# Clearing a row buffer in two halves and reordering the first loads of an attention and feed-forward kernel

## What is computed

```
for t in range(S):
    cur = einsum('bhd,bhe->bhde', u * k[t], v[t])
    y[t] = einsum('bhd,bhde->bhe', r[t], state + cur)
    state = w * state + einsum('bhd,bhe->bhde', k[t], v[t])
x = y as (3072 tokens, 384)
h = x @ w_in;  x = (max(h, 0) + alpha * min(h, 0)) @ w_out
h = x @ w_in2; out = (h * tanh(log1p(exp(h)))) @ w_out2
```

## Time and profile before

| | |
|---|---|
| median of 3 runs | 1009.12 us |
| the runs | 1009.12, 1012.5, 1008.62 us |
| the profiled execution | 1010.13 us |
| its span in the trace | 1008.4 us |
| granted TensorE clock, mean | 0.999 of full speed |
| TensorE busy | 979.0 us, 97% of the span |
| VectorE, ScalarE, GpSimd busy | 660.3, 644.3, 374.2 us |

### The profile page before, as it was taken

One profiled execution on the slowest core, in us unless ns is written; L12 is line 12 of the kernel. 1 busy time (PEld: TensorE's weight loads), 2 busy tenths in 40 slices (PEclk: granted clock), 3 DMA queues, 4 the chain that ended last, 5 costly groups with the idle time before them and its releaser, 6 DMA issues.

```text
span 1008.4 us, 24355 instructions
## 1 busy us (share of the span) xinstructions
PE 979.0 (97%) x9476; PEld 801.9 (80%) x9476; DVE 660.3 (65%) x1421; ACT 644.3 (64%) x1456; POOL 374.2 (37%) x663
## 2 busy tenths in 40 slices
PE   4978999999999999999999999999999999999998
PEld 3866788888888887888878888888888888888886
DVE  6776776655655665665553345877768777777775
ACT  6765665545555555545554667877777777787775
POOL 7878776666656666655620340000000000000000
PEclk9999999999999999999999999999999999999999
DMA  5234341211121121111103232000000000000000
GB/s 171 65 84 130 108 123 51 86 45 45 46 78 47 53 76 44 51 55 61 29 6 134 90 94 95 32 1 32 32 32 7 26 31 0 0 31 0 32 1 31
DMA packets 24614, 54.33 MB, mean 54 GB/s; under 512 B 4928, under 2 KB 12736, under 8 KB 24512
## 3 DMA queue, kind: packets, MB, share of 16 engines
q1 hardware_dynamic: 22640, 43.43, 14.5%
q10 hardware_dynamic: 1872, 9.49, 2.3%
HBM read 41.10 MB, written 9.44 MB: 50 GB/s over the span
## 4 chain that ended last, share of the span: by engine, by line
PE 93%; DVE 2%; DMA 2%; SPq 1%; ACT 1%; issue 1%; POOL 0%; DVEq 0%; ACTq 0%; POOLq 0%
PE acc L979 41%; PE hid L963 29%; PE lev L963 10%; PE lev L1022 8%; PE tok L1040 2%; PE tok L1045 2%; DMA arena<-rk_t 2%; DVE scores L569 1%; SPq L304 1%; PE lev L1006 1%; ACT scores L819 0%; PE hid L1022 0%; PE acc L1040 0%; DVE w_lo L654 0%; DVE x_parts L587 0%
## 5 line engine op out<-in xcount | busy, mean ns | idle before, releaser
L963 PE MATMUL hid<-x_parts,w_hi 128*128 128x512 f32 x864 | 291.1, 391 | 3.6 <-DVE w_lo L654 3.6
L979 PE MATMUL acc<-g_hi,w_hi 128*128 128x512 f32 x576 | 233.2, 405 | 0.0
L979 PE MATMUL acc<-g_hi,w_lo 128*128 128x512 f32 x576 | 224.8, 390 | 0.0
L963 PEld LDWEIGHTS hid<-x_parts,w_hi 128*128 128x128 f32 x864 | 163.0, 189 | 38.1 <-issue 4.0
L660 DVE SCALAR_TENSOR_TENSOR hid<-relu_neg,neg_slope,hid 128x512 f32<-128x512 f32 x96 | 72.5, 756 | 170.0 <-ACT hid L856 169.8
L855 ACT ACTIVATE relu_neg<-hid 128x512 f32<-128x512 f32 x96 | 57.2, 596 | 197.6 <-PE hid L963 197.6
L963 PE MATMUL hid<-x_parts,w_lo 128*128 128x512 f32 x432 | 168.8, 391 | 0.0
L979 PE MATMUL acc<-g_lo,w_hi 128*128 128x512 f32 x576 | 162.1, 390 | 0.0
L569 DVE COPY_PREDICATED scores<-mask,lev 128x128 f32<-128x128 int8 x425 | 152.1, 358 | 11.5 <-issue 0.4
L293 POOL TENSOR_TENSOR arena<-arena,power_rev 112x128 f32<-112x128 f32 x228 | 94.4, 448 | 141.8 <-PE lev L1022 141.0
L979 PEld LDWEIGHTS acc<-g_hi,w_hi 128*128 128x128 f32 x576 | 108.0, 188 | 23.8 <-issue 0.2
(11 more groups left out here) (91 smaller groups left out, 1393.1 us busy)
## 6 DMA issues: line engine op xcount, KB each, us to landing
w_raw<-weights SPq DMA_DIRECT2D x32, 384.0 KB, 3.6
arena<-rkv SPq DMA_DIRECT2D x24, 384.0 KB, 3.5
arena<-rk_t SPq DMA_DIRECT2D x48, 192.0 KB, 3.5
arena<-rkv SPq DMA_DIRECT2D x24, 192.0 KB, 2.7
x_dram<-result ACTq DMA_DIRECT2D x6, 768.0 KB, 3.5
arena<-x_dram SPq DMA_DIRECT2D x6, 768.0 KB, 4.3
out<-result ACTq DMA_DIRECT2D x6, 768.0 KB, 3.3
x_parts<-y SPq DMA_DIRECT2D x141, 16.0 KB, 1.9
```

The costliest lines, as they stand in the source:

```text
L963: last = nc.tensor.matmul(to[:, 0:TILE], w[:, j, kt * P:(kt + 1) * P], x[:, par, kt], start=x is x_hi and w is w_hi and kt == 0, stop=x is ...
L979: last = nc.tensor.matmul(acc[d][:, 0:TILE], w[:, j, cols], g[:, j % RING], start=j == 0 and g is g_hi and w is w_hi, stop=j == STEPS - 1 ...
```

## The change

GpSimd's single memset of `rk_rows` becomes two, one for each parity's half, and each counts `zero_pool` up by one. SyncE issues the first chunk's rows directly behind the decay, after the first half is cleared; the by-token rows of chunk 0 come behind them, then `v`, the bonus, and the by-token rows of chunk 1. After a wait for the second half come the rows of chunk 1, and only then the first weight slot and the slope. Chunk 1's `v` and the weight slots 1 and 2 follow as before. ScalarE's wait for `power_split` counts one more.

```
@@ block.sync
             for q in range(2):
                 sp.dma_start(w_pow[HALF * q:HALF * q + D, 0], decay[q]).then_inc(s_decay, 16)
-            load_rk(0)
-            sp.dma_start(bonus_tok[:], bonus.partition_broadcast(P)).then_inc(s_small, 16)
             sp.wait_ge(zero_pool, 1)
             load_rows(0)
+            load_rk(0)
             load_v(0)
+            sp.dma_start(bonus_tok[:], bonus.partition_broadcast(P)).then_inc(s_small, 16)
+            load_rk(1)
+            sp.wait_ge(zero_pool, 2)
+            load_rows(1)
             load_weights(0)
             sp.dma_start(neg_slope[:], slope).then_inc(s_small, 16)
-            load_rk(1)
-            load_rows(1)
             load_v(1)
             load_weights(1)
             load_weights(2)
@@ block.gpsimd
-            nc.gpsimd.memset(rk_rows[:], 0.0).then_inc(zero_pool, 1)
+            for par in range(2):
+                nc.gpsimd.memset(rk_rows[:, par], 0.0).then_inc(zero_pool, 1)
@@ block.scalar
-                act.wait_ge(zero_pool, 2)
+                act.wait_ge(zero_pool, 3)
```

## The result

| | before | changed |
|---|---|---|
| median, 22 runs each | 1009.12 us | 1011.88 us |
| lowest and highest | 1006.96 to 1012.5 | 1009.62 to 1015.43 |
| profiled execution, its span | 1010.13, 1008.4 us | 1013.85, 1012.1 us |

The ratio is 1.0022, with a 95% interval of 1.0011 to 1.0032: +2.2 us (1.1 to 3.2) on 1009; the two medians are 2.8 us apart. That is slower beyond the interval and inside the 0.5% that the prediction called the same.

A forecast was written before the change was run, and what follows sets the result against it. TensorE, busy 97% of the span, bounds the kernel, so only the dense work's start matters. Earlier rows (-0.8) and the later slope (+2.3) add 1.5 us to 1009.12: 1010.6 us, own range 1009.6 to 1011.8, wider 1007.6 to 1013.0.

The forecast's parts named there:

- The rows come earlier: Head of the chain: chunk 0's rows issued 0.94 us sooner, so L443 could start 0.8 us sooner, at about 11.8.
- The slope comes later: GpSimd's L443 waits for the slope, landing at 14.0, and starts at 14.1, 2.3 us after the 11.8 otherwise possible.
- the same set of transfers: Loads up to chunk 1's second row load plus the slope; the set's landing at 14.0 was taken for the slope.
- the first rival: Slope lands before 11.8, so L443 does not wait and only the gain of 0.8 us is left: 1008.3 us; 15%.
- The bounds beside the landing: Slope's landing at L443: at earliest 9.0 us from bytes ahead at 392 GB/s, at latest 15.8 with a further 384 KB.
- Weight slot 0 costs nothing: ScalarE's L780 wants it at 16.4 after the shift; it lands at about 13.8; without that cover it costs its lateness.
- The sum: Chain head to end: -0.8 for the rows, +2.3 for the slope, +1.5 us in all, a median of 1010.6 us.
- the wider one: Range for the measured time including the faster rival and the scatter of three runs: 1007.6 to 1013.0 us.
- I find no place between 14 and 76 us at which the chain waits for something with a time of its own: Chain from the first diagonal to the dense work: a shift at 14 us should reach 76 us and the end in full.
- L443 late and the dense work still at 76 us: Sign in the changed profile that would show the forecast wrong and the second rival right; 77.6 us was forecast for dense work.
- the second rival: No net change: slope late, but the delay ends before 76 us in the loop over the first chunks; 1009.1 us; 17%.

The follow-up runs named there:

- e3: Kernel before with the memset of `rk_rows` in two halves, all waits for both, load order unchanged: 1009.15 us, ratio 0.9995.
- e4: The changed kernel run again without an edit: 1011.86 us, ratio 1.0017.
- e1: Changed kernel with the slope issued directly behind the bonus: 1009.45 us, ratio 1.0001.
- e2: Kernel before with only the slope's load moved behind both row loads of chunk 1: 1010.98 us, ratio 1.0016.
- e10: Changed kernel, same load order, slope on its own semaphore; GpSimd waits for the bonus only, VectorE's use of the slope moved behind unit 4: 1009.62 us, ratio 1.0005.
- e6: Kernel before with an extra GpSimd memset of 2304 elements a partition directly ahead of L443, no transfer moved: 1011.32 us, ratio 1.0019.
- e7: Kernel before with an extra GpSimd memset of 3840 elements a partition directly ahead of L443, no transfer moved: 1012.08 us, ratio 1.003.
- e8: e1 with ScalarE's split of weight slot 0 moved from ahead of unit 0's copies to ahead of unit 2's: 1009.32 us, ratio 0.9999.
- e9: Changed kernel with loads ordered rows 0, token rows 0, bonus, slope, v 0, weight slot 0, token rows 1, rows 1: 1008.9 us, ratio 0.9991.
- e5: Kernel before run again without an edit, under its own label: 1010.28 us, ratio 1.0007.

## Why the prediction was right, and where it was not

**The rows come earlier: right.** L293 at 7.85, no wait for a load, TensorE's transposes next, L441 0.8 us ahead. The landing, 5.9, lies in the 5 to 6.5 taken. The two memsets took 1.84 us for 1.80, and e3 shows that nothing follows from them.

**The slope comes later: right, by the same set of transfers.** Landing taken 14.0, found 14.2, and 14.6 in e4, so the first rival (there before 11.8) falls; L443 taken 14.1, found 14.33 and 14.71; idle time taken 2.3, found 2.57. e1 (take the lateness away: 2.4 us less), e2 (add it to the kernel before: 1.7 us more) and e10 (take only the wait away) pin the cost on this one wait. The bounds beside the landing rest on a wrong reading. The 2.36 MB of the set are not all that the DMA engines moved between 3 and 14 us: the trace of the kernel before has 3.07 MB there, a mean of 280 GB/s, so some 0.7 MB of the loads issued behind the set was moved before the set was complete. A further 384 KB would then be 1.4 us and not 1.8, and a landing can't be had from the bytes issued ahead alone.

**Weight slot 0 costs nothing: right only under its cover.** It landed at 14.0 (13.8 taken) and was wanted at 16.60. Without the slope's wait it cost what the prediction said it would, what it is late, in e1 (14.58 for 14.12, 0.46 us of the chain), where it landed at 14.56. In e10, with the changed kernel's order, it landed at 14.0 and cost nothing.

**The sum: mis-sized.** +1.5 was forecast and +2.2 measured (1.1 to 3.2), in the interval but below its middle; the median, 1011.88, lies 0.1 us above the forecast's own range of 1009.6 to 1011.8 and inside the wider one. The term off is the delay at L443. I took 12.61 as its start before. The old order of loads has it, or the memset in its place, at 12.61, 12.60, 12.17 (e3), 11.86 (e6) and 11.87 (e7), a mean of 12.2, and the changed kernel has 14.33 and 14.71, a mean of 14.5. Against the 11.84 of e1 the gain for the early rows is 0.4 us and not 0.8, and the slope's price 2.7 and not 2.3: 2.3 us together. At the full clock the changed kernel stands at 1010.65 in its first runs and 1011.59 in e4, 2.1 and 3.0 above the 1008.5 of the kernel before.

**"I find no place between 14 and 76 us at which the chain waits for something with a time of its own": wrong.** There are two, chunk 3's row load and the long hole-copy issue, worth up to 1.2 and 0.7 us. They made the dense work start at 76.0 in both profiles, where 77.6 was forecast for the changed one. The prediction's own check, "L443 late and the dense work still at 76 us", would have chosen the second rival, and wrongly: over the executions the shift is passed on (e2, e6, e7). That rival falls for the time and holds for this pair of profiles.

**The clock** was not in the prediction. It made the pair of spans 3.7 us apart (1012.1, where 1009.9 was forecast); it appears in both kernels, and at the full clock the difference stays.

**What stays open:** why one hole copy's issue in each six takes 0.9 to 2.0 us and the others mostly 0.6; why the changed kernel is 0.9 us faster at the full clock in its first executions than in e4; what decides whether the clock falls at 92 us in a given execution, since the idle stretches before it are alike; whether e8 or e9 is faster than the kernel before by the 0.4 to 0.6 us that they show at the full clock, which two sets of the kernel before can differ by as well.

## What to carry to other kernels

When a load is put ahead of others, look first at what is now last, and at every semaphore that it shares: here an 8 KB load that nobody needed early held up the kernel, because it was counted together with one that was needed. A transfer's landing was forecast here to 0.2 and 0.6 us in two profiles from the transfer that closed the same set before; the bytes ahead of it gave only wide bounds. A shift of a microsecond or two is not to be read from one profile of each kernel: compare executions at the same granted clock, and look for the transfers and issues whose own time varies between the shift and the end.

## What the runs showed of the hardware that I had not expected

- TensorE's clock fell to 1.2 GHz at about 91 to 95 us in six of the twelve profiles, the kernel before once with and once without, after the same two idle stretches of 0.6 and 1.4 us. A long stretch costs 3.7 us, a shorter one about 1.
- The issue of a copy within the on-chip memory took SyncE 0.59 us, and one in each set of six 0.9 to 2.0 us (0.92 in e3, 1.96 in e9).
- Loads issued behind a set of loads were in part moved before that set was complete: 3.07 MB between 3 and 14 us, of which the set is 2.36 MB.
- The same load, issued by 3.32 us, landed 5.2 us (e7), 5.6 us (e3) or 6.0 us (before, e5) later in the same order of loads, which moved GpSimd's work by 0.75 us.
